# First group of a fused recurrence and expert kernel: an earlier second transpose, later third-chunk scores and products, and a re-ordered VectorE list

## The reference

```
# 1: linear recurrence with per-feature decay, 8 heads of 48
y[t]  = r[t] @ (state + u*k[t] (x) v[t]);  state = w * state + k[t] (x) v[t]
# 2: layer norm, then a two-layer perceptron 384 -> 1536 -> 384, with residual
x2 = x + relu(layernorm(x) @ w_ch1) @ w_ch2
# 3: eight experts, one per token, chosen by a gate (sticky from token to token)
out[t] = p[e] * (relu(x2[t] @ w1[e]) @ w2[e])
```

## Time and profile before

| quantity | value |
|---|---|
| median of 3 runs | 385.69 us (385.58 to 385.90) |
| the profiled execution | 384.97 us, span 383.1 us |
| TensorE busy | 372.5 us, 97% of the span |
| VectorE, ScalarE, GpSimd busy | 285.5, 155.4 and 137.5 us |
| share of TensorE in the chain that ended last | 91% |

### The profile page before, as it was taken

How to read it: one execution, slowest core, us unless ns; L and a number is a source line. 1 busy time by engine, 2 the same in 40 slices (tenths; PEclk the granted TensorE clock), 3 DMA queues, 4 the chain that set the end, 5 groups by cost and what they waited for, 6 DMA issues and landing times.

```text
span 383.1 us, 8871 instructions
## 1 busy us (share of the span) xinstructions
PE 372.5 (97%) x3056; PEld 338.6 (88%) x3056; DVE 285.5 (75%) x630; ACT 155.4 (41%) x281; POOL 137.5 (36%) x114
## 2 busy tenths in 40 slices
PE   8999999999999999999999999999999999999993
PEld 6899999999999999999999656789999999999982
DVE  7799899988897997868878568798546764647440
ACT  6556313212322221241441254368525852555530
POOL 2999784911760570100004006303332233223231
PEclk9999999999999999999999999999999999999998
DMA  7999603302500330500038484799874287111011
GB/s 218 328 329 285 212 22 113 112 21 67 157 36 21 110 110 26 181 3 22 21 97 286 134 308 144 264 372 305 301 277 151 87 277 284 43 34 43 26 45 43
DMA packets 32923, 56.67 MB, mean 148 GB/s; under 512 B 3294, under 2 KB 20484, under 8 KB 32753
## 3 DMA queue, kind: packets, MB, share of 16 engines
q1 hardware_dynamic: 30576, 49.84, 39.9%
q0 software_dynamic: 2304, 6.30, 5.3%
HBM read 51.41 MB, written 5.51 MB: 149 GB/s over the span
## 4 chain that ended last, share of the span: by engine, by line
PE 91%; DVE 5%; issue 1%; DMA 1%; ACT 1%; POOL 0%; SPq 0%; POOLq 0%; DVEq 0%; ACTq 0%
PE bank L1039 18%; PE bank L935 7%; PE bank L937 7%; PE bank L936 7%; PE bank L1367 5%; PE bank L1339 5%; PE bank L1375 5%; PE bank L1371 5%; PE bank L1343 5%; PE bank L1346 5%; PE bank L1356 3%; PE bank L953 3%; PE bank L1268 3%; PE bank L1245 3%; PE bank L984 2%; PE bank L974 2%
## 5 line engine op out<-in xcount | busy, mean ns | idle before, releaser
L1039 PE MATMUL bank<-xnT_hi,parts 128*128 128x256 f32 x432 | 65.3, 287 | 0.5 <-ACT xnT_hi L726 0.2
L1677 DVE SCALAR_TENSOR_TENSOR stage<-stage 128x384 f32<-128x384 f32 x81 | 60.7, 791 | 0.1
L1039 PEld LDWEIGHTS bank<-xnT_hi,parts 128*128 128x128 f32 x432 | 56.6, 191 | 2.0 <-ACT xnT_hi L726 0.5
L733 ACT ACTIVATE parts<-bank 128x512 fp32r<-128x512 f32 x36 | 21.5, 597 | 90.6 <-PE bank L1039 90.5
L667 POOL DMA_INDIRECT out_y<-late x14 | 20.5, 1462 | 93.9 <-DVE late L1964 93.9
L935 PE MATMUL bank<-parts 128*128 128x384 f32 x144 | 49.3, 342 | 0.0
L937 PE MATMUL bank<-parts 128*128 128x384 f32 x144 | 48.2, 335 | 0.0
L936 PE MATMUL bank<-parts 128*128 128x384 f32 x144 | 48.2, 334 | 0.0
L813 ACT ACTIVATE parts<-stage (+1 forms) x32 | 46.2, 1485 | 0.4 <-DMA stage<-in_w 0.4
L1933 DVE TENSOR_TENSOR parts<-stage,parts x24 | 41.1, 1755 | 4.9 <-ACT parts L813 4.2
L1039 PE MATMUL bank<-xnT_lo,parts 128*128 128x256 f32 x216 | 37.4, 282 | 0.0
(11 more groups left out here) (257 smaller groups left out, 732.6 us busy)
## 6 DMA issues: line engine op xcount, KB each, us to landing
stage<-in_w SPq DMA_DIRECT2D x36, 768.0 KB, 6.7
stage<-in_w_ch SPq DMA_DIRECT2D x6, 768.0 KB, 7.8
arena<-in_k_t SPq DMA_DIRECT2D x12, 224.0 KB, 3.2
arena<-in_r_t SPq DMA_DIRECT2D x12, 224.0 KB, 3.1
arena<-in_v_rows SPq DMA_DIRECT2D x12, 192.0 KB, 3.9
arena<-in_k_rows SPq DMA_DIRECT2D x12, 192.0 KB, 3.2
x_rows<-stage SPq DMA_DIRECT2D x12, 192.0 KB, 1.9
arena<-in_r_rows SPq DMA_DIRECT2D x10, 192.0 KB, 3.3
```

The source lines that it names most:

```text
L733: act.activation(hT_hi[:, 2 * q:2 * q + 2, :].rearrange("p a t -> p (a t)"), bk[6 + q % 2][:], ACT.Relu).then_inc(h_hi_ready, 1)
L1039: mm = pe.matmul(acc, w[:, k, at], x[:, k, :], start=start and k == 0, stop=stop and k == KD - 1, skip_group_check=first and q == 0)
L1677: dve.scalar_tensor_tensor(spent[n % NSPENT], x2[t % 2], 1.0, wgr[e], ALU.mult, ALU.mult, accum_out=lg[:, t, e:e + 1]).then_inc(s_spent, 1)
```

## The change

On TensorE the transposes of tile 1 come directly behind those of tile 0, ahead of both gains, and two `keep_warm` matmuls are gone. ScalarE takes tile 1's high part before it rounds the second half of piece 0. In group 0 TensorE does pairs 0, 1 and 2 before chunk 2's scores, pair 3 before `chunk(2)` and pair 4 before chunk 3's scores. VectorE's list is put in another order to go with that.

```diff
--- before.py
+++ after.py
@@ -792,9 +792,9 @@
             round_first(0)
             for u in range(2):
                 first_centred(u)
-            round_first(1)
             act.wait_ge(s_ng, 1)
             turned_tile(0, 1)
+            round_first(1)
             round_piece(1)
             act.wait_ge(s_wc, 1)
             group(0)
@@ -1129,11 +1129,11 @@
 
                 pe.wait_ge(xnT_hi_ready, g * 2 + 2)
                 if first:
-                    hidden(g, range(0, 2))
+                    hidden(g, range(0, 3))
                     scores(g * 2 + 2, 0, bk[0:2])
-                    hidden(g, range(2, 3))
+                    hidden(g, range(3, 4))
                     chunk(g * 2 + 2, 0, n_lg, ends)
-                    hidden(g, range(3, 5))
+                    hidden(g, range(4, 5))
                     scores(g * 2 + 3, 1, bk[0:2])
                     hidden(g, range(5, NHP))
                     chunk(g * 2 + 3, 1, n_lg, ends)
@@ -1168,11 +1168,10 @@
             keep_warm(5)
             pe.wait_ge(coef_ready, 2)
             turn_tile(0, 0)
+            turn_tile(0, 1)
             pe.wait_ge(s_endS, 1)
             gain(0, 0, bk[3])
-            turn_tile(0, 1)
             gain(1, 1, bk[2])
-            keep_warm(1)
             group(0)
             pe.wait_ge(s_gw, 16)
             with pe.Fori(1, NG - 2) as g:
@@ -1441,9 +1440,11 @@
                 dve.wait_ge(s_pair, NP_)
                 dve.tensor_tensor(rkT[0], kT[0], rT[0], ALU.mult).then_inc(rkT_ready, 1)
 
-            def third_decays():
+            def third_r_decays():
                 dve.wait_ge(s_turned[0], T_FIRST[0] + T_LOADS)
                 dve.tensor_tensor(rT[0], rT[0], w_r, ALU.mult).then_inc(rdec_ready, 1)
+
+            def third_k_decays():
                 dve.tensor_tensor(kT[0], kT[0], w_k, ALU.mult).then_inc(kdec_ready, 1)
 
             def first_coefs(c, bank):
@@ -1640,26 +1641,27 @@
 
             def first_group():
                 hidden(0, range(0, 1))
+                third_k_decays()
+                hidden(0, range(1, 2))
                 new_state(0, 0, bk[3])
-                hidden(0, range(1, 2))
+                hidden(0, range(2, 3))
                 masked(2, bk[0:2], scT[0])
                 new_state(1, 1, bk[2])
                 rest_of_piece(2)
-                hidden(0, range(2, 3))
+                coefs(2, 0)
+                hidden(0, range(3, 4))
                 new_state(2, 0, bk[3])
-                coefs(2, 0)
                 first_stats()
                 means(0)
-                hidden(0, range(3, 4))
+                sums(2, 0, bk[4])
                 rest_of_piece(3)
-                sums(2, 0, bk[4])
+                hidden(0, range(4, 5))
                 masked(3, bk[0:2], scT[0])
                 moments(2, 0)
-                hidden(0, range(4, 5))
+                coefs(3, 1)
+                hidden(0, range(5, NHP))
                 new_state(3, 1, bk[3])
-                coefs(3, 1)
                 rest_of_piece(5)
-                hidden(0, range(5, NHP))
                 rows_of(3, 1, bk[4])
                 means(1)
                 scales(0)
@@ -1740,7 +1742,7 @@
             first_rows(1, bk[5])
             first_turned()
             turned(0, range(1, 2))
-            third_decays()
+            third_r_decays()
             first_group()
             for g in range(1, NG - 2):
                 group(g)
```

## The result

| quantity | before | changed |
|---|---|---|
| median of 7 runs each, same chip | 385.90 us | 388.22 us |
| ratio, 95% interval | | 1.0060 (1.0041 to 1.0079) |
| the profiled execution, its span | 384.97, 383.1 us | 388.22, 386.3 us |
| first half of group 0 ends (first L935) | 37.60 | 40.27 |
| chunk 4's scores (L953) | 50.97 | 53.65 |

The change makes the kernel slower by 0.6%, 2.3 us in the medians; one of the seven changed runs, at 394.39 us, was disturbed, and the median of the other six is 387.84, 1.9 us above the kernel before. The last three lines of the table tell where the time goes: the shift is 2.67 us when group 0's first half ends, 2.68 at chunk 4's scores, and 2.69 at the end of the program. All of it is made in the first 24 us of group 0, and no later wait takes any of it up.

What follows compares the result with a forecast made beforehand. TensorE was taken to bound the kernel, with VectorE as full in group 0; -0.34 head, -0.21 and -0.48 old waits, +1.43 and +2.33 new ones, 0.1 rounding gave +2.8 us on 385.69: 388.5, range 386.7 to 389.5.

Steps and rivals of the forecast that it cites:

- The forecast case: Whole kernel: the forecast as worked out, +2.8 us to a median of 388.5 us, given a chance of 0.75.
- Any idle time it puts on VectorE's list before `masked(3)` goes straight to TensorE: Group 0: VectorE has no gap from 17.52 to 35.41, as full as TensorE, so idle time there delays TensorE.
- The gap for the relu of pair 2: VectorE ahead of `masked(2)`: idles 1.86 us because ScalarE's relu of pair 2 stands behind `decay(2)`, which waits for `new_state(0)`.
- the 0.7 of the earlier trace: Behind group 0 TensorE's longest wait is 0.7 us, so a shift made in group 0 reaches the end nearly whole.
- rival 3: TensorE's clock falls in the new stalls of 1.43 and 2.33 us: some +4, 392.5 us; chance 0.03.
- the first decay: VectorE in group 0: first decay runs 0.17 us earlier, 17.35 to 19.1, before 0.8 us idle for pair 0's relu.
- pair 1 has room for that too: Head: GpSimd starts the low part of piece 0's second half 0.2 us later, at no cost to TensorE's pair 1.
- pair 4's wait costs nothing: TensorE in pair 4: piece 2's low part is done at 30.76, wanted at 30.82, so the wait costs nothing.
- The TensorE sum: Group 0: 16.41 plus pairs 0, 1, 2, scores(2) and pair 3 gives 26.84, when TensorE wants gain(2).
- GpSimd is busy in the whole stretch, so it stands beside them wherever they lie: Group 0, argument against rival 1: VectorE's long operations stay slow beside GpSimd's work even when moved.
- rival 1: VectorE's long operations in group 0 shrink, set free of GpSimd, decay 0.61: +1.2 us, 386.9 us; chance 0.12.
- Rival 2: VectorE never late, `masked(3)` done by 34.5, only TensorE's sum counts: 0.94 us sooner, 384.8 us; chance 0.06.

Runs made afterwards that it cites:

- 7: Kernel before plus a needless 1024-column write on VectorE directly ahead of `masked(3)`; ratio 1.0038, first half ends 38.78.
- 8: Kernel before plus the same needless 1024-column VectorE write directly behind `masked(3)`; ratio 1.0021, first half ends 37.78.
- experiment 6: Changed kernel with ScalarE's relu of pair 2 ahead of `decay(2)` in group 0 alone; ratio 1.0026, first half ends 39.52.
- experiment 2: Changed kernel with its old head put back, so group 0's new order alone; ratio 1.0034, first half ends 38.73.
- experiment 9: Changed kernel with GpSimd's k decay of chunk 3 held until VectorE has done piece 2's subtraction; ratio 1.0051, first half ends 39.41.
- experiment 3: Kernel before with the new head and TensorE's new group 0 order, but VectorE's old list; ratio 1.0015, first half ends 40.31.
- 1: Kernel before with the change's new head alone, group 0 in its old order; ratio 0.9989, first half ends 37.93.

## Why the prediction was right

388.5 was predicted, 388.22 measured; for the half's end +2.82, and +2.67. The forecast case came true and no rival did. Step by step (the waits are reckoned here as the prediction did, from the start of the last pair plus 2.26; the profile's brackets, which count to the end of the last matmul, have 0.69 and 1.68):

| step | predicted | measured |
|---|---|---|
| pair 0 starts | 16.41 | 16.57 (over the runs 16.43 to 16.73 with the new head, 16.67 to 16.85 with the old) |
| VectorE idle for the relu of pair 0 | 0.8 | 1.69 |
| VectorE idle for the relu of pair 1 | 0 | 0.42 |
| second decay | 2.0 | 1.78 |
| VectorE idle for the relu of pair 2 | 1.86 | 1.72 |
| TensorE ready for gain(2) | 26.84 | 27.28 |
| gain(2), its wait | 28.27, 1.43 | 28.13, 0.85 |
| TensorE held in pair 4 | 0 | 0.5 |
| gain(3), its wait | 38.30, 2.33 | 38.18, 1.84 |
| half ends | 40.42 | 40.27 |

**The mechanism holds.** "Any idle time it puts on VectorE's list before `masked(3)` goes straight to TensorE" is measured by itself in 7 and 8 (1.05 us in, 1.00 out). The gap for the relu of pair 2 stands where it was put, with 1.72 for 1.86, and experiment 6 shows that `decay(2)` makes it. gain(2) and gain(3) both start when VectorE is done. The shift runs to the end unchanged, as the 0.7 of the earlier trace rows had it. And TensorE's clock was not touched by stalls of 0.7 and 1.7 us: in these windows of the changed kernel, chunk(2) behind the first stall, chunk(3) behind the second and what follows it, it is 1.00 (columns as in the earlier trace rows), so rival 3 did not occur:

```profile
28.13:30.22 2.09, 2.09 (x64) 2.04 (x64) 2.09 (x1) 1.56 (x3) 2.09 (x2) 1.00 1.05 363
...
38.18:40.27 2.09, 2.09 (x65) 2.04 (x65) 2.08 (x5) 0.00 (x0) 2.09 (x2) 1.00 0.96 335
40.27:42.30 2.03, 2.03 (x14) 2.03 (x12) 1.97 (x3) 0.00 (x0) 0.11 (x1) 1.00 0.93 381
```

**Three terms were mis-sized, all about GpSimd.** The first is the first decay, taken to keep its 1.82: it took 0.68, so VectorE was free at 18.03, and the gap for the relu of pair 0, which ScalarE sets, was 1.69 and not 0.8. Work that became shorter only made the wait longer. The second is the sentence "pair 1 has room for that too": GpSimd's half piece started not 0.2 but 0.4 us later (17.32 against 16.94) and took 2.41, as VectorE's decay had gone first, and pair 1 waited 0.44. I had reckoned ScalarE's and TensorE's lists there and not looked up when GpSimd's three halves end. The third is "pair 4's wait costs nothing": piece 2's subtraction took 2.83 and not 2.52, and from the start of pair 4 (30.22) to chunk 3's scores (32.99) there are 2.77 us instead of 2.26.

The last two held TensorE in places that I had at nothing, and they were paid differently. Pair 4's 0.5 cost nothing in the end: VectorE sets gain(3) in any case, so the time only came out of the wait there, and 2.33 became 1.84. Pair 1's wait did cost: the relu of pair 1 came at 21.88, VectorE, free at 22.1, stood 0.42 us for it, and with this low part `new_state(0)`, the relu of pair 2 and gain(2) came as much later. Experiments 2 and 9 show it: where pair 1 waited little or not, that low part began 0.61 and 0.42 sooner (21.91 and 22.10 against 22.52), and gain(2) by the same 0.61 and 0.42. Up to gain(2) the late one was thus not VectorE's list alone, but the chain from GpSimd over TensorE's pair 1 and ScalarE's relu to VectorE. The wait is hidden in the total only because the second decay was shorter than reckoned: the low part of pair 1 was forecast for 22.48. A forecast by the engine that is late does not depend on where another waits only as long as that wait does not reach back to it.

The TensorE sum has two more errors that nearly cancel: pair 0 took 2.25 and not the 2.57 of the earlier trace rows, and pair 1 took 2.86 and not 2.25.

**What was right by luck.** VectorE's lengths were carried over from before, one by one, and argued with "GpSimd is busy in the whole stretch, so it stands beside them wherever they lie". That is false: GpSimd was busy, yet the lengths changed by -1.14, -0.56, +0.31 and -0.34. What decides is who comes first and how much the other has left. Up to `new_state(1)` VectorE's waits for relus took up the shorter decays, and it ended within 0.1 of the forecast (28.11 against 28.21); behind it piece 2's +0.31 and piece 3's -0.34 cancelled. That is luck: experiment 2 has the same order in group 0 and ends at +1.13, which is all but rival 1's +1.2 (it was given 0.12; its 1.755 for the subtractions comes out in 2 as 1.76 and 1.82, its second decay of 0.61 as 1.20). The rival should have had a larger chance, and the range, which reached down to it, was right to do so. Rival 2 (TensorE keeps the lead) had no run near it: `masked(3)` would have had to end by 34.5 and with TensorE's new order it never ended before 36.54 (experiment 2).

The Trainium skill (SBUF — State Buffer, section SBUF: two separate sides) says that VectorE and GpSimd share a pair of ports that is locked, not divided: whichever starts first, a VectorE operation with two SBUF inputs or a GpSimd one that reads SBUF, holds it for the whole instruction, and the other stands still. These traces agree: 1.76 beside 2.87, 2.83 beside 1.29, and 2.02 in experiment 9. The prediction cited only a page's word of contention, with which such lengths could not be worked out.

## What to carry to other kernels

First ask which engine is late, and follow its list with the gaps in it: a reordering that frees TensorE's own path brings nothing when it puts an idle gap on the engine that TensorE will meet two waits later. Where VectorE and GpSimd both work on operands in SBUF (VectorE with two of them), do not carry a length over from a trace when its start moves: take its time alone, and add what is left of the other engine's instruction at that moment, both ways. And judge a gain of 0.3 us at the head only at the end: here it was given back 17 and 32 us later, by a GpSimd product that met VectorE and by a late transfer.

## What the runs showed of the hardware that I had not expected

**Turns are taken whole, and a few hundredths of a microsecond decide.** VectorE's 112 x 512 product takes 0.68 alone and 1.20 to 2.34 behind a GpSimd instruction; its 1536-column subtraction 1.75 to 3.31; GpSimd's 128 x 384 products 0.8 to 1.0 alone and up to 2.5 behind VectorE, its 112 x 512 one 1.28 or 2.8. Whether VectorE began 0.03 us ahead of GpSimd (experiment 2) or 0.07 behind it (the changed kernel) moved its subtraction by 1.07 us. (Starts on GpSimd are recorded roughly: at its first decay VectorE stands at 17.35, 0.03 behind GpSimd's row, and still went first.) VectorE's operations with one input in PSUM kept their time everywhere (L1568 and its like 0.66 to 0.69 us, L1466 1.22 to 1.29 for two), GpSimd busy or not.

**It makes parts of a change not add up.** Head alone +0.33, group alone +1.13, both +2.67: in these traces 1.2 us belong to neither part, but to the moments at which the two engines meet. The timed ratios (0.9989, 1.0034, 1.0060) point the same way, but are too wide to show it.

**What stays open.** The order of VectorE's list has no clean price of its own (experiment 3 had a late DMA, and its times and its trace disagree). Most kernels have one trace, and how the turns fall in their other runs is not known. And it is open why chunk 2's k arrives late in 3 and 6 but not in 1 or in the changed kernel; it is issued at 8.2 to 8.5 us in all of them.
